# Attention in tiles of 128 tokens with q stationary, and key-value products per head in 64-column pieces

## The reference, cut to what matters

```python
# q, k, v: (4, 8, 576, 64) f32; g_norm: (64,)
kv  = np.einsum('bhsd,bhse->bhde', k, v)
out = np.einsum('bhsd,bhde->bhse', q, kv)
rms = np.sqrt(np.mean(out * out, axis=-1, keepdims=True) + 1e-06)
x   = out / rms * g_norm            # then (b, s, h*d): 2304 tokens x 512
# layer 1: d_ff 2048
h = x @ w_in
g = h * np.tanh(softplus(h))
x = g @ w_out
# layer 2: d_ff 1024
h  = x @ w2_in
e  = np.exp(h - h.max(-1)); solu = h * e / (e.sum(-1) + 1e-9)
ln = (solu - mean(solu)) / np.sqrt(var(solu) + 1e-06) * g_ln
return ln @ w2_out
```

## Time and profile before

| | us |
|---|---|
| median of 3 runs | 720.53 (719.54 to 722.01) |
| profiled execution, its own time | 719.26 |
| its span | 716.6 |
| attention stage with `up(0)` and `up(1)`, to the first `down` | 98.67 |
| from there to the end | 617.9 |
| busy in the span: PE, DVE, ACT, POOL | 684.8, 275.5, 242.9, 102.2 |

### The profile page before, as it was taken

How to read it: one execution, slowest core, us unless ns; L and a number is a source line. 1 busy time by engine, 2 the same in 40 slices (tenths; PEclk the granted TensorE clock), 3 DMA queues, 4 the chain that set the end, 5 groups by cost and what they waited for, 6 DMA issues and landing times.

```text
span 716.6 us, 8343 instructions
## 1 busy us (share of the span) xinstructions
PE 684.8 (96%) x3216; PEld 562.1 (78%) x3216; DVE 275.5 (38%) x534; ACT 242.9 (34%) x482; POOL 102.2 (14%) x72
## 2 busy tenths in 40 slices
PE   7887669999999999999999999999899999999998
PEld 5765458888888889988888888888688888888886
DVE  1999952111311122131111411214854545454542
ACT  2765542222222223222222222223443434343432
POOL 0364975000000000000000001706500000000000
PEclk9998989999999999999999999999999999999999
DMA  8982333000000000000000000301100000000001
GB/s 277 343 294 89 106 109 108 1 1 0 1 1 0 1 0 2 1 0 1 1 1 0 1 0 1 118 0 31 33 31 16 29 16 31 15 30 16 30 16 44
DMA packets 12551, 32.12 MB, mean 45 GB/s; under 512 B 1760, under 2 KB 3040, under 8 KB 12512
## 3 DMA queue, kind: packets, MB, share of 16 engines
q1 hardware_dynamic: 12512, 31.60, 13.2%
HBM read 26.87 MB, written 4.72 MB: 44 GB/s over the span
## 4 chain that ended last, share of the span: by engine, by line
PE 87%; DVE 6%; issue 5%; DMA 1%; ACT 0%; SPq 0%; DVEq 0%
PE bank L298 23%; PE bank L300 23%; PE bank L299 23%; PE bank L412 4%; PE bank L413 4%; PE bank L414 4%; PE bank L428 2%; PE bank L312 2%; DVE cv L656 1%; DVE yv L649 1%; PE bank L379 1%; DMA kvt<-kv_pairs 1%; DVE cv L661 1%; PE bank L321 1%; DVE kv L638 0%
## 5 line engine op out<-in xcount | busy, mean ns | idle before, releaser
L676 DVE TENSOR_TENSOR g_lo<-gb,g_hi 128x512 fp32r<-128x512 f32 (+1 forms) x80 | 57.9, 724 | 297.1 <-ACT g_hi L512 297.1
L505 ACT ACTIVATE gb<-bank 128x512 f32<-128x512 f32 (+1 forms) x80 | 44.3, 554 | 292.5 <-PE bank L300 292.5
L298 PE MATMUL bank<-g_hi,wout_hi 128*128 128x512 f32 (+1 forms) x320 | 118.7, 371 | 5.5 <-DVE g_lo L676 5.5
L298 PE MATMUL bank<-xs_hi,win_hi 128*128 128x512 f32 (+1 forms) x320 | 121.0, 378 | 2.7 <-DVE yv L649 2.4
L300 PE MATMUL bank<-xs_hi,win_lo 128*128 128x512 f32 (+1 forms) x320 | 119.6, 374 | 0.0
L299 PE MATMUL bank<-xs_lo,win_hi 128*128 128x512 f32 (+1 forms) x320 | 119.3, 373 | 0.0
L299 PE MATMUL bank<-g_lo,wout_hi 128*128 128x512 f32 (+1 forms) x320 | 118.5, 370 | 0.0
L300 PE MATMUL bank<-g_hi,wout_lo 128*128 128x512 f32 (+1 forms) x320 | 118.4, 370 | 0.0
L298 PEld LDWEIGHTS bank<-g_hi,wout_hi 128*128 128x128 f32 x320 | 60.5, 189 | 16.9 <-issue 5.9
L298 PEld LDWEIGHTS bank<-xs_hi,win_hi 128*128 128x128 f32 x320 | 60.5, 189 | 15.6 <-POOL win_lo L256 2.9
L300 PEld LDWEIGHTS bank<-xs_hi,win_lo 128*128 128x128 f32 x320 | 60.4, 189 | 11.6
(11 more groups left out here) (70 smaller groups left out, 850.5 us busy)
## 6 DMA issues: line engine op xcount, KB each, us to landing
kvt<-kv_pairs SPq DMA_DIRECT2D x16, 512.0 KB, 10.5
stage<-w_in SPq DMA_DIRECT2D x12, 512.0 KB, 3.6
stage<-w_out SPq DMA_DIRECT2D x12, 512.0 KB, 3.5
qs<-qt SPq DMA_DIRECT2D x16, 288.0 KB, 10.2
out<-ot SPq DMA_DIRECT2D x18, 256.0 KB, 2.0
kvt<-kv_pairs SPq DMA_DIRECT2D x16, 64.0 KB, 11.4
ones<-ones_in SPq DMA_DIRECT2D x1, 64.0 KB, 4.7
ident<-ident_in SPq DMA_DIRECT2D x1, 64.0 KB, 3.4
```

The lines of the kernel that those rows point to most:

```text
L298: nc.tensor.matmul(dst, w_hi, x_hi, start=start, stop=False)
L505: nc.scalar.activation(gb[s % 2][:, 0:n], h_ps[s % 4][:, 0:n], ACT.Mish).then_inc(g_done, 1)
L676: vec.tensor_tensor(g_lo[s % 2][:, 0:n], gb[s % 2][:, 0:n], g_hi[s % 2][:, 0:n], ALU.subtract).then_inc(glo_done, 1)
```

## The change

The attention stage is rewritten. It now goes over 18 tiles `t` of 128 tokens for all 8 heads at once, across the borders of the batches (tile 4 and tile 13 hold tokens of two batches). `STARTS` is 0, 4, 9, 13: the tile at which each batch begins; `ENDS` is 5, 9, 14, 18.

- `pair_kv(b, c)`: each product of 128 columns becomes two of 64 columns, one per head, whose outputs lie in partitions 0 to 63 and 64 to 127. All four chunks of a batch share one bank; two banks take turns. `kv_blocks(b)` copies a whole batch with two copies of 64x256.
- `attend(t)`: q is stationary and `kvb` moves, four products of 128 columns for a tile (for tiles 4 and 13 four for each of the two batches). The result is tokens by features. The product with the matrix of 1/64 is gone.
- `square(t)` on ACT is 128x512. DVE sums each head's squares (`tensor_reduce`, 128x512 to 128x8), ACT takes the reciprocal root of 128x8, and the Newton step is four DVE operations of 128x8. One DVE operation of 128x512 reads PSUM and the factors and writes `xk`.
- `turn_x(t)`: four PE transposes bring the tile back to features by tokens, and ACT `keep_x(t)` writes `X` from PSUM with g_norm as its scale.
- At the first tile of each later batch PE does the four `pair_kv` of the batch with three transposes between them, and DVE finishes the tile before.
- The hi and lo parts of the first block of `X` move from POOL to DVE (`x_parts(0, ...)`, eight operations, half at tile 9 and half at tile 13).
- Inputs: kv and q of a batch come in one DMA each (batch 0's kv still in chunks), `ident` comes at the start, `ones` is gone. POOL's unit out0 now waits for tile 13's `attend`, and unit out4 for the last `X`.

```diff
-            def pair_kv(g, chunks=range(SC + 1)):
...
+            def pair_kv(b, c):
+                n = b % 2
...
+                    if b >= 2:
+                        pe.wait_ge(kv_sb, 2 * (b - 1))
+                for a in range(SC + 1):
                     rows = P if a < SC else SR
-                    last = nc.tensor.matmul(kv_ps[:, c, :], kvt[n][0:rows, c, a, 0:P], kvt[n][0:rows, c, a, P:2 * P],
-                                            start=(a == 0), stop=(a == SC))
+                    for e in range(0, P, D):
+                        last = nc.tensor.matmul(kv_ps[n][e:e + D, c, :], kvt[n][0:rows, c, a, e:e + D],
+                                                kvt[n][0:rows, c, a, P + e:P + e + D], start=(a == 0), stop=(a == SC))
...
+            def attend(t):
+                if t >= 4:
+                    pe.wait_ge(att_y, t - 3)
+                for b, s, n, r in segments(t):
+                    if s <= P:
+                        pe.wait_ge(kv_sb, 2 * (b + 1))
+                        pe.wait_ge(q_in[b], 16)
+                    for c in range(KC):
+                        last = nc.tensor.matmul(o_ps[t % 4][r:r + n, c * P:(c + 1) * P], qs[b % 2][:, c, s:s + n],
+                                                kvb[b % 2][:, c, :], start=True, stop=True)
+                last.then_inc(att_mm, 1)
+
+            def turn_x(t):
+                pe.wait_ge(att_y, t + 1)
+                if t >= 2:
+                    pe.wait_ge(att_x, t - 1)
+                for c in range(KC):
+                    last = nc.tensor.transpose(x_ps[t % 2][:, c * P:(c + 1) * P], xk[t % 3][:, c * P:(c + 1) * P],
+                                               ident[:, :])
+                last.then_inc(att_t, 1)
...
+            for t in range(NT):
+                if t in STARTS[1:]:
+                    for c in range(KC):
+                        pair_kv(STARTS.index(t), c)
+                        if c < XL:
+                            turn_x(t - XL + c)
+                attend(t)
+                if t - XL >= opened(t):
+                    if t == XL:
+                        pe.wait_ge(ident_dma, 16)
+                    turn_x(t - XL)
+            up(0, (0, 1))
+            turn_x(NT - 3)
+            up(0, (2, 3))
+            turn_x(NT - 2)
             up(1, (0, 1))
-            mean_square(NU - 1)
+            turn_x(NT - 1)
             up(1, (2, 3))
...
+            for t in range(NT):                      # ACT
+                square(t)
+                if t - 1 >= opened(t):
+                    first_root(t - 1)
+                if t - XL >= opened(t):
+                    keep_x(t - XL)
+                if t + 1 in STARTS:
+                    first_root(t)
+                    for n in range(XL):
+                        keep_x(t + 1 - XL + n)
+            first_root(NT - 1)
             nc.scalar.preload_act_table_set("mish_and_others")
...
+            def mean_square(t):                      # DVE
+                dve.wait_ge(att_sq, t + 1)
...
+                vec.tensor_reduce(ms[t % 3][:, :], by_head(sq[t % 2][:, :]), AX_X, ALU.add).then_inc(att_ms, 1)
+                dve.wait_ge(att_ms, t + 1)
...
+                vec.tensor_scalar(msa[t % 3][:, :], ms[t % 3][:, :], 1.0 / D, RMS_EPS, ALU.mult, ALU.add
+                                  ).then_inc(att_a, 1)
+            def scale_out(t):
...
+                vec.tensor_tensor(rsq[:, :], rt[t % 3][:, :], rt[t % 3][:, :], ALU.mult).then_inc(att_r2, 1)
+                dve.wait_ge(att_r2, t + 1)
...
+                vec.scalar_tensor_tensor(out=rc[:, :], in0=msa[t % 3][:, :], scalar=-0.5, in1=rsq[:, :],
+                                         op0=ALU.mult, op1=ALU.mult).then_inc(att_c, 1)
+                dve.wait_ge(att_c, t + 1)
...
+                vec.scalar_tensor_tensor(out=rf[:, :], in0=rc[:, :], scalar=1.5, in1=rt[t % 3][:, :],
+                                         op0=ALU.add, op1=ALU.mult).then_inc(att_r, 1)
+                dve.wait_ge(att_r, t + 1)
...
+                vec.tensor_tensor(by_head(xk[t % 3][:, :]), by_head(o_ps[t % 4]),
+                                  rf[:, :].unsqueeze(2).to_broadcast([P, H, D]), ALU.mult).then_inc(att_y, 1)
...
+            kv_blocks(0)
+            for t in range(NT):
+                mean_square(t)
+                if t - 1 >= opened(t):
+                    scale_out(t - 1)
+                if t + 1 in STARTS:
+                    scale_out(t)
+                    if t + 1 == STARTS[2]:
+                        x_parts(0, (0, 1))
+                    if t + 1 == STARTS[3]:
+                        x_parts(0, (2, 3))
+                    kv_blocks(STARTS.index(t + 1))
+            scale_out(NT - 1)
...
-                        pool.wait_ge(kv_mm, NP)      # POOL, unit out0
-                        pool.wait_ge(att_mm, NU - UB)
-                    if n == 3:
-                        pool.wait_ge(att_x, NU)
+                        pool.wait_ge(kv_mm, B)
+                        pool.wait_ge(att_mm, ENDS[B - 2])
+                    if n == 4:
+                        pool.wait_ge(att_mm, NT)
+                        pool.wait_ge(att_x, NT)
```

More of the change, by code:

```diff
@@ L19 @@
 NC2 = F2 // P
-SH = S // 2
 SC = S // P
@@ L31, with segments, opened @@
 JU = NJ // U1
[L32 to L41, removed]
+XL = 3
+def segments(t):
+    found, at = [], t * P
+    while at < (t + 1) * P:
+        b, s = divmod(at, S)
+        n = min(S - s, (t + 1) * P - at)
+        found.append((b, s, n, at - t * P))
+        at += n
+    return found
+STARTS = [max(0, b * S // P) for b in range(B)]
+ENDS = [((b + 1) * S + P - 1) // P for b in range(B)]
+def opened(t):
+    return max(n for n in STARTS if n <= t)
 ORDER = ([("in", n) for n in range(U1 // 2 + 1)]
@@ L72, in build @@
         tiny = sb("tiny", [P, 2, 16])
+        ident = sb("ident", [P, P])
+        ms = [sb(f"ms{n}", [P, H]) for n in range(3)]
+        msa = [sb(f"msa{n}", [P, H]) for n in range(3)]
+        rt = [sb(f"rt{n}", [P, H]) for n in range(3)]
+        rsq = sb("rsq", [P, H])
+        rc = sb("rc", [P, H])
+        rf = sb("rf", [P, H])
         ra = ExitStack()
@@ L315, in pair_kv @@
+                if c == KC - 1:
                     last.then_inc(kv_mm, 1)
[L317 to L320, removed]
-                nc.tensor.matmul(m_ps[u % 3], ones[:, :], sq[u % 2][:, :], start=True, stop=True).then_inc(ms_mm, 1)
+            def attend(t):
[9 more added lines that the diff above has]
+                last.then_inc(att_mm, 1)
@@ L518, in keep_acc @@
                     nc.scalar.activation(X[:, m, t0:t0 + n], acc[:, m, 0:n], ACT.Copy).then_inc(x2a_done, 1)
-            square(0)
-            square(1)
-            for u in range(NU):
-                ln_mean_square(u)
-                if u + 2 < NU:
-                    square(u + 2)
-                first_root(u)
-                root_square(u)
-            nc.scalar.preload_act_table_set("mish_and_others")
-            for s in range(NS - 1):
+            for t in range(NT):
[9 more added lines that the diff above has]
+            first_root(NT - 1)
+            nc.scalar.preload_act_table_set("mish_and_others")
+            keep_x(NT - 3)
+            keep_x(NT - 2)
+            gate(0)
+            g_part(0)
+            keep_x(NT - 1)
+            for s in range(1, NS - 1):
                 if s % NJ == 1 and s > NJ:
@@ L618, in _, with x_parts @@
             vec = nc.vector
-            def x_parts(i):
+            def x_parts(i, chunks=range(KC)):
                 t0, n = BLOCKS[i]
-                dve.wait_ge(h_done, i * NJ)
-                for c in range(KC):
+                if i == 0:
+                    dve.wait_ge(att_x, n // P)
+                else:
+                    dve.wait_ge(h_done, i * NJ)
+                for c in chunks:
                     vec.tensor_copy(xs_hi[:, c, 0:n], X[:, c, t0:t0 + n]).then_inc(xs_hi_done, 1)
```

247 lines of the change are left out of this document (92 added, 155 removed).

## The result

The changed kernel takes 708.08 us (median of 4 runs, 707.38 to 708.36) where the kernel before, in runs beside it, takes 720.03; the ratio is 0.983, 95% interval 0.9806 to 0.9854. The forecast was 712 with a range of 699 to 723. The time is close and the direction right, but that closeness is luck: the first `down` came 5.6 us later than I had it, and the rest of the kernel, which I had left untouched, became 7.5 us shorter.

What follows compares the result with a forecast made beforehand. DVE waiting for POOL was taken to bound the stage before the first `down`, PE everything after. First `down` 8.2 us earlier gives span 708.4, plus 2.7 around it 711.1, median 1.3 above, so 712 us; range 699 to 723.

Steps and rivals of the forecast that it cites:

- PE is the bound behind the first `down`, and the change touches nothing there: From 98.67 us to the end: PE busy 611.55 of 617.93 us at full clock, so this stretch stays the same.
- two of its own signs: Signs of a wrong prediction: tile 13's attend ending outside 60 to 70 us; first `down` to end not 618 within 1.
- the slow clock is there in both: First products of layer 1: slow clock before and after the change, since PE idles ahead of it; no difference counted.
- DVE waits for POOL's instructions: Attention stage: DVE operations with two SBUF inputs, or such tensor-scalar ones, wait for POOL's running instruction; `factor` 2.47 against 0.30 us.
- Small operations pass in pairs, 3.6 us a tile: Tiles beside POOL: two small DVE operations pass at one POOL instruction's end, 3.6 us a tile; chance 0.42, time 712.
- The rival in which each waits for one POOL instruction, 7.1 us a tile: Tiles beside POOL: every small operation waits for one instruction; first `down` 98.2, time 720, no change; chance 0.26.
- the one in which none waits: Rival for tiles beside POOL: small operations don't take the port; first `down` near 68.5, -30, time 690; chance 0.09.
- Free pace of 2.0 us a tile: DVE in the new attention stage while POOL rests: 2.0 us a tile, 36 for 18, bounds 1.7 and 2.4.
- Narrow passes: PE's 64-column passes in the key-value products: between 0.055 and 0.11 us at full clock, taken as 0.08; 25.6 us for 320.
- The timetable: Attention stage laid out by tiles and batch borders of 4.9 us each: first reduction 15.3, last xk 88, first `down` 90.5.
- the slower rival: Batch borders longer because PE's clock falls: +4.1 a border, +12 for three, first `down` 102.7, time 724.5; chance 0.23.
- one term: The attention stage ahead of the first `down`: it starts at 90.5 instead of 98.67 us, -8.2.

Runs made afterwards that it cites:

- e1: Kernel before with one unused tile of 896 bytes behind `tiny`, putting the weight tiles where the changed kernel has them; 715.61 us, ratio 0.992.
- e2: Changed kernel with an unused tile of 128 bytes behind `rf`, putting the weight tiles 1024 bytes above their place in the kernel before; 717.01 us, ratio 0.9938.
- e10: e6 with an unused tile of 128 bytes ahead of `xs_hi`, so the x tiles and the weight tiles all move by 128; 693.14 us, ratio 0.9609.
- e8: Kernel before with weight tiles shifted by 896 bytes and POOL waiting before unit in5 for the last X; 706.92 us, ratio 0.9798.
- e5: Changed kernel with POOL waiting before weight unit in5 for the last xk; 698.67 us, ratio 0.9686.
- e6: Changed kernel with weight units reordered (in0, in1, out0, in2, out1 and so on) and POOL waiting before in2 for the last xk; 692.58 us, ratio 0.9599.
- e11: e6 with 256 bytes more behind `rf`, so the weight tiles are shifted by 1152 bytes; 693.76 us, ratio 0.9624.
- e12: e6 without the explicit preload of the gate's table, and with gate(0) and g_part(0) ahead of keep_x(16); 693.75 us, ratio 0.9621.

## Why the prediction came out as it did

- **PE is the bound behind the first `down`, and the change touches nothing there: wrong.** This is the step that failed. I said that the prediction is wrong if that stretch isn't 618 us within 1; it was 610.4. So by two of its own signs (the other is tile 13, below) the prediction is wrong, though its time and range hold. The diff's tile list moved the weights against the x tiles, and that alone is worth -2.55 + 0.32 - 2.65 - 2.37 = -7.25 us. e1 and e2 show it from both sides, e10 shows that it is the distance of the two tiles. Another part is the clock at the first products of layer 1, in the kernel before and in the changed one:

```profile
98.67 0.76 PE L298 MATMUL bank<-g_hi,wout_hi 128*128 128x512 f32 x1 [5.51 <-DVE g_lo L676]
99.23 0.63 PE L299 MATMUL bank<-g_lo,wout_hi 128*128 128x512 f32 x1
...
96.10 0.47 PE L297 MATMUL bank<-g_hi,wout_hi 128*128 128x512 f32 x1
96.41 0.40 PE L298 MATMUL bank<-g_lo,wout_hi 128*128 128x512 f32 x1
```

PE had paused 5.51 us ahead of them in the one and 0.11 in the other. The three kernels with the old stage (before, e1, e8) all have a pause of 4.7 to 6.1 us there and 0.63 us a product, the other ten at most 1.8 us and 0.40. I had said that the slow clock is there in both, and that was 1.5 us here, 2.1 between e8 and e5. Against these two stands +1.28 us in the passage to layer 2, where the clock fell in the changed kernel's profile and not in that of the kernel before; why, I don't know.
- **DVE waits for POOL's instructions: right**, and it is what bounded the stage. e5 and e6 take the waits away by moving POOL's work, and the times fall by 9.4 and 15.5 us.
- **Small operations pass in pairs, 3.6 us a tile: right.** Four intervals of xk, 4.6, 3.5, 3.5 and 3.5; from the first reduction of tile 13 to the end of the last xk 22.4 us, forecast 22.3. The rival in which each waits for one POOL instruction, 7.1 us a tile, is out, and so is the one in which none waits. The Trainium skill's page "SBUF — State Buffer" (section "SBUF: two separate sides") is borne out in what it says on who waits for whom. It is borne out too in that the one which starts first holds the ports: rf at 86.03 passes ahead of POOL's 86.07, rf at 57.71 waits behind POOL's 57.70. So the page's rule allows the pairs, and I was wrong to say that it gives the rival of 7.1 us.
- **Free pace of 2.0 us a tile: right**, 2.00 in the changed kernel before POOL starts and in e5.
- **Narrow passes: too dear.** 0.08 taken, 0.044 measured at full clock and 0.074 at the low one; even my least, 0.055, was too much. Beside the drain that the Trainium skill names (page "TensorEngine Tiling (Array Packing)", section "Key Properties") stands 0.09 us for the one kind of change measured here, from transposes to narrow products.
- **The timetable: 5.6 us short.** First reduction 17.8 and not 15.3, since q of batch 0 let attend start at 14.98 and not at 13.7, and attend ran at the low clock (32 passes in 5.75 us) (+2.5); tiles 0 to 3 +0.8; border 1, 5.2 for 4.9; border 2, 7.8 for 4.9; border 3, 6.0 for 4.9; the two stretches of tiles between were 1.4 shorter than taken (what I named for tiles 9 to 12, one free and three locked, adds up to 12.8 and not to the 14.4 that I took), the last stretch and the tail 0.5. The longer borders, which I had given to the slower rival, made 4.3 of the 12 us that it had. Nearly all of it is the clock: from the last xk to the copies the changed kernel takes 2.0 us more at border 2 (clock 0.50) and 1.2 more at border 3 (0.76) than e11 at 0.98 and 1.00, and from attend to the first reduction of tile 9 it takes 2.7 us at 0.50 where e10 takes 1.8 at 1.00. Tile 13's attend was due at 64.7 and POOL's out0 began at 71.00, outside the 60 to 70 I allowed.

So the forecast had a gain of 8.2 us out of one term. Measured are 2.6 from that term and 7.5 from three that I had at nothing: 7.25 by the place of the tiles, 1.5 by the clock at the first `down`, less 1.3 in the passage. That the two errors nearly cancel is luck.

## What to carry to other kernels

Read what POOL runs beside DVE before pricing a DVE stage: an operation with two SBUF inputs, or a tensor-scalar one like `factor` and msa, cost the rest of POOL's running instruction here, and 128x8 waited as long as 128x288 (rc 2.33 us, `factor` 2.47). Moving POOL's work behind the stage was worth more (15 us) than rewriting the stage (2.6 us, 4 with the warmer start; 6.6 against e1, whose weights lie where the changed kernel has them). When a change adds or removes a tile, compare the pace of untouched products by kind before and after; if it moved, vary the distance of the two operands with an unused tile ahead of blaming anything else. A pause of PE can cost twice, in itself and in the clock behind it: here pauses of 2.4 and 2.5 us were followed by a stretch at the low clock, while one of 2.8 us (e5, at 75.77) and five of 3.0 to 3.4 were not. And before an edit is credited with an earlier start, compare the stretches ahead of the edit too.

## What the runs showed that I had not expected

- float32r products of 512 columns start 227 ns apart when their two operand tiles lie 0 or 256 bytes apart modulo 512, and 233 ns when 128; at 256 columns it is 120.0 and 118.8 ns. In this kernel 128 bytes of unused SBUF move the whole time by over 5 us.
- The same pause of PE, 3.0 to 3.4 us at the same place, leaves the clock high in five profiles and low in eight, 1.6 us apart and 2.8 in one case.
- An explicit load of the gate's table did not spare the load ahead of the first gate: both of 1.28 us were recorded in e6, one remained in e12.
